# Attention and routing on 128 partitions with a fifth group of 64, in place of 96 partitions with six tokens

## The reference

```
q, k, v: (8 batches, 8 heads, 576 tokens, 64)
k_p, v_p = mean of 8 neighbouring tokens of k, v        # 72 keys
attn = softmax(q k_p^T / 8);  x = attn v_p              # rows: (4608 tokens, 512)
logits = x w_gate;  noisy = logits + log1p(exp(x w_noise)) * noise   # 8 experts
top2 of noisy, softmax of the two = weights
y = sum over the two experts e of weight * relu(x w1[e]) w2[e]       # 512 -> 1024 -> 512
out = (h - tanh(h)) w_out,  h = y w_in                               # 512 -> 2048 -> 512
```

## Time and profile before

| | us |
|---|---|
| median of 3 runs | 1929.85 (1929.79 to 1931.75) |
| profiled execution, its time | 1930.99 |
| its span, first to last instruction | 1929.3 |
| TensorE busy in the span | 1886.9 |
| VectorE busy | 997.1 |
| ScalarE busy | 817.8 |
| GpSimd busy | 518.1 |

### The profile page before, as it was taken

The page is one execution under the profiler, slowest core; times in us unless marked ns, Lnnn a source line. Parts: engine busy times, 40 slices in busy tenths (PEclk is TensorE's granted clock), DMA queues, the critical chain, the costliest instruction groups (busy, mean ns, idle before and its releaser), DMA issues.

```text
span 1929.3 us, 35482 instructions
## 1 busy us (share of the span) xinstructions
PE 1886.9 (98%) x13064; PEld 1719.3 (89%) x13065; DVE 997.1 (52%) x1920; ACT 817.8 (42%) x1719; POOL 518.1 (27%) x507
## 2 busy tenths in 40 slices
PE   7999899999999999999999999999999999999999
PEld 6988888898999999999989888999999999999998
DVE  5888733413122131312313177666677777776665
ACT  5988623324222232322323254444444444444444
POOL 2254552122111121211122332222322222222222
PEclk9999899999999999999999999999999999999999
DMA  8987534314113141321314120001100000100000
GB/s 194 234 189 166 133 82 142 131 44 150 46 65 109 43 138 47 114 71 45 129 48 143 71 77 34 33 33 50 48 33 33 33 33 33 33 33 33 33 33 22
DMA packets 94360, 152.22 MB, mean 79 GB/s; under 512 B 18912, under 2 KB 62048, under 8 KB 91488
## 3 DMA queue, kind: packets, MB, share of 16 engines
q1 hardware_dynamic: 70304, 100.24, 16.6%
q0 software_dynamic: 24000, 51.26, 9.8%
HBM read 110.54 MB, written 40.40 MB: 78 GB/s over the span
## 4 chain that ended last, share of the span: by engine, by line
PE 88%; DMA 4%; DVE 3%; issue 2%; POOL 2%; ACT 1%; ACTq 0%; DVEq 0%; SPq 0%; POOLq 0%
PE banks L844 14%; PE banks L843 14%; PE banks L842 14%; PE banks L833 13%; PE banks L835 13%; PE banks L834 13%; DMA slot_row<-row_w,slot_w 3%; PE banks L823 3%; POOL slot_row L538 1%; PE banks L708 1%; PE banks L731 1%; POOL k_raw L502 0%; DVE w_lo L1401 0%; PE banks L717 0%; PE banks L869 0%
## 5 line engine op out<-in xcount | busy, mean ns | idle before, releaser
L833 PE MATMUL banks<-x_hi,w_hi 128*128 128x256 f32 x2304 | 637.7, 277 | 6.1 <-DVE x_lo L1420 4.0
L835 PE MATMUL banks<-x_hi,w_lo 128*128 128x256 f32 x2304 | 637.2, 277 | 0.0
L834 PE MATMUL banks<-x_lo,w_hi 128*128 128x256 f32 x2304 | 637.0, 276 | 0.0
L842 PE MATMUL banks<-w_hi,h_hi 128*128 128x512 f32 x1184 | 467.3, 395 | 3.0 <-DVE h_lo L1502 3.0
L844 PE MATMUL banks<-w_hi,h_lo 128*128 128x512 f32 x1184 | 466.0, 394 | 0.0
L843 PE MATMUL banks<-w_lo,h_hi 128*128 128x512 f32 x1184 | 463.1, 391 | 0.0
L833 PEld LDWEIGHTS banks<-x_hi,w_hi 128*128 128x128 f32 x2304 | 433.5, 188 | 9.1 <-DVE x_lo L1420 4.5
L834 PEld LDWEIGHTS banks<-x_lo,w_hi 128*128 128x128 f32 x2304 | 433.3, 188 | 2.5
L835 PEld LDWEIGHTS banks<-x_hi,w_lo 128*128 128x128 f32 x2304 | 433.2, 188 | 0.0
L671 POOL TENSOR_SCALAR large<-u_sq 128x512 uint8<-128x512 f32 x144 | 222.4, 1545 | 568.7 <-ACT u_sq L1153 302.0
L1427 DVE SCALAR_TENSOR_TENSOR h_lo<-banks,h_hi 128x512 fp32r<-128x512 f32 x144 | 99.6, 692 | 362.5 <-ACT h_hi L1082 351.4
(11 more groups left out here) (167 smaller groups left out, 2049.9 us busy)
## 6 DMA issues: line engine op xcount, KB each, us to landing
w_raw<-in_moe_w SPq DMA_DIRECT2D x32, 1024.0 KB, 5.0
y<-y_rows SPq DMA_DIRECT2D x17, 1024.0 KB, 5.2
q_sb<-in_q SPq DMA_DIRECT2D x32, 288.0 KB, 6.3
x_rows<-x_sb SPq DMA_DIRECT2D x32, 288.0 KB, 4.7
out_x<-y_sb SPq DMA_DIRECT2D x36, 256.0 KB, 2.1
k_raw<-in_k SPq DMA_DIRECT2D x16, 288.0 KB, 4.8
v_raw<-in_v SPq DMA_DIRECT2D x16, 288.0 KB, 6.4
w_raw<-in_moe_w_in SPq DMA_DIRECT2D x4, 1024.0 KB, 4.8
```

The lines of the kernel that those rows point to most:

```text
L833: pe.matmul(part, hi, x_hi[:, c, :], start=(c == 0), stop=False)
L834: pe.matmul(part, hi, x_lo[:, c, :], start=False, stop=False)
L835: mm = pe.matmul(part, lo, x_hi[:, c, :], start=False, stop=(c == NC - 1))
L842: pe.matmul(p_y[m][:, :], hi, w_hi[par][:, o:o + DM], start=(j == 0), stop=False)
```

## The change

Tokens lie on 128 partitions, four consecutive ones each (512 tokens, `FULL`), and a fifth group holds the last 64 tokens on 64 partitions. Everything on 96 partitions with six tokens becomes five groups: two score matmuls of 144 columns and one of 72 (64 partitions of input) in place of three; five transpositions, exponentials and value matmuls in place of six; two transpositions of Q a head, and for every second head one of 64 rows that holds both heads of the pair. K and V stay on 96 partitions. Q, x, slots and noise each go by two DMAs, the full part and the half part. Slots and weights have the pair of experts innermost, so that the row number of a slot is its place in the list, and `row_w` comes from one iota. The weights have one array. Six memsets fill what the fifth group leaves open.

```
-    TT = 6
-    TP = S // TT
+    TP = 128
+    TG = S // TP
+    TH = S - TG * TP
+    TT = TG + 1
+    FULL = TG * TP
...
-                sp.dma_start(q_sb[:, p, :, :], q_v[:, bass.ds(b * H + 2 * p, 2), :]).then_inc(q_in[p], 16)
+                u = b * H + 2 * p
+                sp.dma_start(q_sb[:, p, 0:2 * TG * D].rearrange("p (r n) -> p r n", r=2), q_full[:, u:u + 2, :]).then_inc(q_in[p], 16)
+                sp.dma_start(q_sb[0:TH, p, 2 * TG * D:2 * TT * D].rearrange("p (r n) -> p r n", r=2), q_half[:, u:u + 2, :]).then_inc(q_in[p], 16)
...
+                sp.dma_start(x_v[b, 0:FULL, cols].rearrange("(p t) n -> p t n", t=TG), x_sb[:, 0:TG, p, GW:GW + 2 * D]).then_inc(x_out[p], 16)
+                sp.dma_start(x_v[b, FULL:S, cols], x_sb[0:TH, TG, p, GW:GW + 2 * D]).then_inc(x_out[p], 16)
...
-            pool.iota(row_all[:, :, :], pattern=[[2 * S, B], [1, 2], [2, TT]], base=2 * PAD, channel_multiplier=2 * TT
-                      ).then_inc(iotas, 1)
+            pool.iota(row_w[:, :, :], pattern=[[2 * S, B], [1, WAY]], base=2 * PAD, channel_multiplier=WAY).then_inc(iotas, 1)
...
-                for t in range(HALF):
-                    mm = pe.matmul(p_s[u % 2][0:TP, t * 2 * KEYS:(t + 1) * 2 * KEYS], qT[:, t * TP:(t + 1) * TP],
-                                   kT[:, u, :], start=True, stop=True)
+                for t in range(TG // 2):
+                    pe.matmul(p_s[u % 2][:, t * 2 * KEYS:(t + 1) * 2 * KEYS], qT[:, t * TP:(t + 1) * TP],
+                              kT[:, u, :], start=True, stop=True)
+                r = u % 2
+                mm = pe.matmul(p_s[u % 2][0:TH, TG * KEYS:TT * KEYS], qT[r * D:(r + 1) * D, FULL // 2:FULL // 2 + TH],
+                               kT[r * D:(r + 1) * D, u, r * KEYS:(r + 1) * KEYS], start=True, stop=True)
...
-                for t in range(TT):
+                for t, n in enumerate(ROWS):
                     cols = slice(t * KEYS, (t + 1) * KEYS)
-                    ins = act.activation(pr[u % 4][:, cols], p_s[u % 2][0:TP, cols], ACT.Exp, bias=mx[u % 2][:, t:t + 1])
+                    ins = act.activation(pr[u % 4][0:n, cols], p_s[u % 2][0:n, cols], ACT.Exp, bias=mx[u % 2][0:n, t:t + 1])
...
+            for i in range(2):
+                dve.memset(p_s[i][TH:TP, TG * KEYS:TT * KEYS], 0.0)
+                dve.memset(p_o[i][TH:TP, TG * VW:TT * VW], 1.0)
+            dve.memset(noise_sb[TH:TP, :, TG, :], 0.0)
+            dve.memset(msum[TH:TP, TG, :], 0.0)
```

More of the change, by code:

```diff
@@ L132, in attention_moe_ffn @@
         slot_f = sb("slot_f", [TP, 2, TT], c=a_ctx)
[L133 to L135 removed]
+        slot_n, slot_r, slot_c = (sb(n, [TP, 2, TT], i32, c=a_ctx) for n in ("slot_n", "slot_r", "slot_c"))
+        slot_i = sb("slot_i", [TP, TT, 2], i32, c=a_ctx)
+        wt = sb("wt", [TP, TT, 2], c=a_ctx)
         row_w = sb("row_w", [128, B, WAY], i32, c=a_ctx)
@@ L161, in attention_moe_ffn @@
         kT = sb("kT", [128, H, 2 * KEYS], c=a_ctx)
-        qT = sb("qT", [128, HT], c=a_ctx)
+        qT = sb("qT", [128, S // 2 + TH // 2], c=a_ctx)
         vp = sb("vp", [128, H, VW], c=a_ctx)
         pr = [sb(f"pr{i}", [TP, TT * KEYS], c=a_ctx) for i in range(4)]
-        pT = [sb(f"pT{i}", [128, 2, HT], c=a_ctx) for i in range(4)]
+        pT = [sb(f"pT{i}", [128, S], c=a_ctx) for i in range(4)]
         a_ctx.close()
@@ L169, in attention_moe_ffn @@
         w_lo.append(sb("w_lo1", [128, WE], f32r))
-        c_w = [sb(f"c_w{i}", [128, TC]) for i in range(2)]
+        c_w = sb("c_w", [128, TC, 2])
         idx_g = sb("idx_g", [128, SUB], i32)
         idx_s = sb("idx_s", [128, SUB], i32)
-        sb("spacer", [128, 80])
+        sb("spacer", [128, 88])
         x_hi = sb("x_hi", [128, NC, NB], f32r)
@@ L193, in attention_moe_ffn @@
         p_s = [banks[:, i, :] for i in (1, 7)]
-        p_a = banks[:, 3:5, :]
+        p_a = banks[:, 3:5, :].rearrange("p a n -> p (a n)")
         p_o = [banks[:, 5 + i, :] for i in range(2)]
@@ L441, in _ @@
             sp.wait_ge(route_out, 32 * B)
-            for i in range(2):
-                sp.dma_start(c_w[i][:, :].rearrange("p (b m) -> p b m", m=SUB),
-                             tok_w[i].rearrange("(b p m) -> p b m", p=128, m=SUB)).then_inc(c_w_in, 16)
+            sp.dma_start(c_w[:, :, :].rearrange("p (b m) i -> p b (m i)", m=SUB),
+                         tok_w.rearrange("(b p m) i -> p b (m i)", p=128, m=SUB)).then_inc(c_w_in, 16)
             def weights(e, nxt, after):
@@ L728, in values @@
                     pe.wait_ge(x_bank, x_use(b, f"vb{u // PAIRS}") + 1)
-                for t in range(TT):
-                    i, o = divmod(t, HALF)
-                    mm = pe.matmul(p_o[u % 2][0:TP, t * VW:(t + 1) * VW], pT[u % 4][:, i, o * TP:(o + 1) * TP],
+                for t, n in enumerate(ROWS):
+                    mm = pe.matmul(p_o[u % 2][0:n, t * VW:(t + 1) * VW], pT[u % 4][:, t * TP:t * TP + n],
                                    vp[:, u, :], start=True, stop=True)
@@ L1348, in part5 @@
                 step(5, b, ins)
-                wait(dve, slot_out, b * 16)
-                step(5, b, dve.scalar_tensor_tensor(out=slot_i[:, :, :], in0=slot_r[:, :, :], scalar=COLS,
+                wait(dve, slot_out, b * 32)
+                step(5, b, dve.scalar_tensor_tensor(out=slot_i[:, :, :].rearrange("p t i -> p i t"), in0=slot_r[:, :, :], scalar=COLS,
                                                     in1=slot_c[:, :, :], op0=ALU.mult, op1=ALU.add))
```

96 lines of the change are left out of this document (48 added, 48 removed).

## The result

| | before | after |
|---|---|---|
| median of four runs, us | 1930.61 (1929.79 to 1931.75) | 2012.76 (1980.90 to 2063.55) |
| ratio | | 1.0269 [1.0244, 1.0294] |
| profiled execution | 1930.99 | 1984.41 |
| its span | 1929.3 | 1982.7 |
| last values matmul of attention | 231.8 | 275.4 |

The change made the kernel slower by 2.7%, outside the predicted range.

A forecast was written before the change was run, and what follows sets the result against it. Attention was taken as bound by TensorE up to 67 us, later by GpSimd's scatter queue, engines nearly level. First scatter -2.0, scatters +1.5, after the table -0.7: -1.2 us from 1929.85 gives 1928.6 us, range 1919 to 1936.

The forecast's parts named there:

- the first price, TensorE at full clock: Attention's matmuls, 31.8 to 67.2 us: new shapes save 0.20 us a head, -2.4 us over twelve heads.
- The sum by proportional prices: The same TensorE saving a head with narrow matmuls priced by columns: -0.26 us, up to -3.1 us over twelve heads.
- The cold stretch: First attention heads, TensorE not yet at full pace: fewer score, values and exponential instructions, 1.2 us shorter together.
- clock rival: First expert block: TensorE waits for the queue, so 10 us more at half clock, +5 us, 1935; chance 0.05.
- The cap: Third block's gather, landing about 281 us: a gain over about 1.5 us needs GpSimd's scatters to be earlier too.
- Setup: Start, before VectorE's first key sum: six new memsets, +0.7 us.
- VectorE: maximum: Attention's maximum and normalising product on fewer elements: -0.15 us a head, -1.4 us a batch with routing.
- ScalarE's exponentials: Attention: six exponentials a head become five, -0.23 us a head, -1.8 us a batch.
- The DMA price: DMA queues in attention: 43 us per MB and 11.4 ns per packet; about 5 us more of all engines.
- the DMA rival: Batch 0's slots and the scatters: extra DMA packets make it slower, +4 to +6 us, 1934 to 1936; chance 0.20.
- the engines were level within 0.66 us: 67 to 219 us: engines and scatter queue nearly level, the queue last by 0.66 us, VectorE's wait for the table.
- the largest rival: Attention: scatters keep up and the engines' saving comes through, a gain of 11 us, 1919; chance 0.30.

The follow-up runs named there:

- the shapes by themselves: TensorE alone, no kernel around it: series of float32 matmuls of one shape, then of two alternating shapes; 111 ns an instruction with 128 stationary columns, 73 with 64, 166 in turn.
- Four in flight: Limit of scatters in flight raised from two to four; 1923.08 us (0.9973) in the kernel before, 1924.93 (0.9981) in the changed kernel padded with late weight loads.
- the padded version: Changed kernel, fifth group padded to 128 rows and columns in all TensorE steps: 1944.74 us (1.0075); with later weight loads also, 1943.29 (1.008).
- the version with rows in order on 96 partitions: Kernel before with only the new slot and weight order, one iota and one weights array, later arrays kept in place; 1928.5 us, ratio 0.999.

## Why the prediction was wrong

**The step that failed** is the first price, TensorE at full clock: "between the column-proportional 62 or 55 ns and the 84 ns at which 81 columns run I take 84, since 81 columns already stay above their proportion". It took the moving columns as the measure of every instruction and the 84 ns as what a narrow one can't get below. The runs put two things in its place. A float32 instruction lasts as long as the longer of its two sides, 0.87 ns for each stationary column or 0.85 for each moving one: eight of the ten values instructions went from 96 to 128 stationary columns and so from 84 to 111 ns, and 8 x 111 + 2 x 73 = 1.03 us is no gain on 1.01, where -0.17 was predicted. The earlier trace rows had shown 109 ns for 128 by 128, which I read as 128 moving columns. And each change between the full array and an instruction of 64 rows or columns stalls, 0.15 us by itself: the values group has two, into its last pair and out of it, and 1.03 + 0.30 is the 1.33 of its chain. A head has six such changes and every second one eight; at 111, 122 and 73 ns its instructions would take 2.45 us, and it takes 3.35, 0.13 us more for each of seven. With keys, values and gates at 0.36 us a head that makes 8 x 3.71 = 29.7 us a batch, the 29.8 measured, where the kernel before took 22.7 to 28.7. This is the 26.6 us of batches 1 to 7. (The sum by proportional prices, -0.26 us a head, comes to -0.29 when it is done again; nothing hangs on it.)

The Trainium skill states both. "TensorE: Matmul & The Clock Gate" (LDWEIGHTS) has a weight load take the stationary columns divided by 1.2 in ns: 107 for 128 and 80 for 96, near the measured 111 and 85. "TensorEngine Tiling (Array Packing)" (Key Properties) says that changing the tiling mode drains TensorE; the runs agree, and put 0.15 us on it. Its configurations have 32, 64 and 128 columns and none of 96, and the turns of 96 with 128 columns were free.

**The cold stretch**, predicted 1.2 us shorter, is most of the other 16.2 us. From 31.9 us, where the kernel before went to full pace, to 60.3 us the changed one works at 5.90 us a head on its chain in place of 3.35, which by estimate costs 28.4 x (1 - 3.35/5.90) = 12 us; the rest is the dearer heads of batch 0. The prediction's clock rival had the right level and the wrong cause and size (+5 us from TensorE's waits for the queue): the half pace lasted 30 us longer with no wait at all. That the order of shapes decides it is shown by the 16 profiles of whole kernels, 62 and 87 us in the two with all the odd shapes and 26 to 35 us in the rest, and by the one fall in the shapes by themselves; what the chip counts is not. Where the rival says that the trace agrees with waits for DMA bringing the half rate, it read too much: the waits of TensorE ahead of its half clock at 192 us and around 223 us were for VectorE where the profile names anything, and none was for a DMA.

**The cap** named in the last term, the third block's gather, did bite: "TensorE waiting for the gather of the third block" was on the list of what would make the prediction wrong. It is worth 6.0 us, and 3.1 with the block after it. Four in flight removed 5.7 of the 8.4 us in the padded version, so most of it there is scatters that wait for each other's landing behind the table load. Why these land more slowly on 128 partitions (12.7 us of waits against 5.2, with a DMA share of 0.01 to 0.05 in both from 240 to 265 us) stays open: the row numbers and their order in the list are the same in the version with rows in order on 96 partitions, which had 4.5.

**What held.** Setup: +0.7 predicted, batch 0 starts 0.8 later (11.4 us; but the nine profiles on 96 partitions start it at 10.5 to 11.4, so this settles nothing). VectorE: maximum 532 and product 575 ns, predicted 525 and 575; ScalarE's exponentials 315 ns and five of them. The DMA price: SyncE's queue in 67 to 275 us moved 25.62 MB in 38537 packets, 1541 us by 43 per MB and 11.4 ns a packet, and took 44.7% of 16 engines, 1488. Nothing of it was on the path, where the DMA rival had put 4 to 6 us. All of this is hidden behind TensorE.

**What bounds before.** That GpSimd's scatters held attention was right: four in flight let it end 7.1 us earlier. That the engines were level within 0.66 us was not; the 0.66 us is the last wait for the table and no measure of what lies behind it. The forecast of the largest rival, that the saving of the engines comes through, could come true only with that limit gone: the padded version then ends attention at 222.1 us, 9.7 us before the kernel before. 96 partitions reach 224.7 in the same way, and 221.7 with the rows in order. From the end of batch 1's first scores the padded version is ahead, 176.1 us beside 180.0 and 180.7, but it starts batch 0 some 2 us later, and two profiles of it with two in flight differ by 5.8 us in this stretch (192.4 and 186.6), so that a gain of the engines there isn't shown. In time nothing is left of the 128 partitions: 1924.93 us, beside 1923.08 and 1922.44.

## What to carry to other kernels

A partition layout that is better for VectorE and ScalarE is paid for on TensorE by every instruction that leaves the common shape. Price a matmul by both of its sides, count the changes between full and 64-wide shapes in the order in which they are issued, and pad the odd group to full width before anything else. A limit on transfers in flight is one number to change, and worth a run before one speeds up the engines behind it. Before two ends of a stage are compared, look in both traces when TensorE came to its full clock: here that alone moved attention's end by 3 us in a kernel whose attention was the same. When a small edit changes the time of code that it doesn't touch, look where the arrays lie.

## What the runs showed of the hardware

- A float32 instruction of TensorE takes 111, 85 and 70 ns with 128, 96 and 64 stationary columns over 81 moving ones, and 122 ns with 144 moving columns whether 96 or 128 are stationary: the longer side sets the pace.
- Arrays 32 or 64 bytes lower in every partition made the same float32r blocks slower: 23.3 to 23.5 us in place of 22.8, and 2.1 to 2.6% of the whole.
- TensorE, busy all the time, went to the half clock at 65.5 us, in a series of alternating shapes, after series of one shape at full clock, and was back at full clock at 137.2 us, in a series of one shape; in the kernel with mixed shapes the full pace came at 62 us in one execution and at 87 us in another of all but the same kernel, and in all others at 26 to 35 us.
- A change of shape costs 0.15 us at full clock, and 0.22 us at half clock: turns of 128 columns over 128 and over 64 rows took 322 ns an instruction there, where one of 128 columns took 213, so 2 x 109.
